# Halves of the second softmax's product with x, eight array places for batches 2 and 3, and two M blocks split ahead of the product

## The reference

```python
def _attn_ref(x, state):                     # x [4, 8, 512, 64], state [4, 8, 32, 64]
    scores = x @ state.T / 8;   a  = softmax(scores);   xread = a @ state
    scores2 = state @ x.T / 8;  a2 = softmax(scores2);  sread = a2 @ x
    return concat([xread, sread], axis=2)    # 544 rows of 64 for each head
# rows to tokens: 4 * 544 = 2176 tokens of 512
def _moe_ref(x, w_in, w_out):                # 512 -> 2048 -> 512
    h = x @ w_in;  return (h * tanh(softplus(h))) @ w_out
def _moe2_ref(x, emb, tau, w1, w2):          # 8 experts, one for each token
    expert = argmax(cosine(x, emb) / tau);  gate = softmax(...)[expert]
    return gate * (relu(x @ w1[expert]) @ w2[expert])
```

## Time and profile before

| | us |
|---|---|
| median of 3 runs | 708.38 |
| lowest and highest | 705.73 and 714.18 |
| the profiled execution, its own time | 706.29 |
| its span | 704.5 |
| TensorE matmul busy in the span | 655.5 |
| VectorE and ScalarE busy | 443.0 and 385.8 |

### The profile page before, as it was taken

How to read it: one execution, slowest core, us unless ns; L and a number is a source line. 1 busy time by engine, 2 the same in 40 slices (tenths; PEclk the granted TensorE clock), 3 DMA queues, 4 the chain that set the end, 5 groups by cost and what they waited for, 6 DMA issues and landing times. The chain is left out here.

```text
span 704.5 us, 12383 instructions
## 1 busy us (share of the span) xinstructions
PE 655.5 (93%) x4142; PEld 512.6 (73%) x4143; DVE 443.0 (63%) x687; ACT 385.8 (55%) x501; POOL 51.6 (7%) x75
## 2 busy tenths in 40 slices
PE   7889979999889999899999888989999999999995
PEld 5667756687667787676588776768888888888884
DVE  6899889888658699576668446472722452272261
ACT  2788679785747787476867333262612442262250
POOL 2000000000200002000002013000001010010101
PEclk9999999999999999999999989999999999999999
DMA  8804443000823002233001612372531261154140
GB/s 245 234 32 132 146 143 120 1 2 25 276 62 120 0 2 86 97 120 120 0 1 61 224 41 81 126 263 91 203 111 45 83 230 34 45 189 139 45 149 5
DMA packets 35350, 72.72 MB, mean 103 GB/s; under 512 B 5699, under 2 KB 5699, under 8 KB 35312
## 3 DMA queue, kind: packets, MB, share of 16 engines
q1 hardware_dynamic: 27728, 56.93, 25.0%
q0 software_dynamic: 3040, 9.13, 3.3%
q10 hardware_dynamic: 4544, 6.14, 3.0%
HBM read 60.92 MB, written 12.16 MB: 104 GB/s over the span
## 5 line engine op out<-in xcount | busy, mean ns | idle before, releaser
L613 PE MATMUL PS<-WH,gh 128*128 128x512 f32 x256 | 103.3, 404 | 0.8 <-DVE gl L1401 0.8
L613 PE MATMUL PS<-WH,gl 128*128 128x512 f32 x256 | 101.0, 395 | 0.0
L613 PE MATMUL PS<-WL,gh 128*128 128x512 f32 x256 | 101.0, 394 | 0.0
L1066 ACT ACTIVATE hh<-PS 128x512 fp32r<-128x512 f32 x42 | 22.9, 595 | 97.5 <-PE PS L717 94.6
L736 PE MATMUL PS<-WH,hh 128*128 (+1 forms) x168 | 69.2, 412 | 3.9 <-DVE hl L1487 2.6
L1477 DVE TENSOR_TENSOR WL<-raw,WH 128x1024 f32 (+1 forms) x48 | 56.3, 1221 | 25.3 <-ACT WH L1046 25.2
L736 PE MATMUL PS<-WH,hl 128*128 (+1 forms) x168 | 67.3, 400 | 0.0
L736 PE MATMUL PS<-WL,hh 128*128 (+1 forms) x168 | 66.9, 398 | 0.0
L1378 DVE SCALAR_TENSOR_TENSOR qq<-ww,PS 128x1024 f32<-128x1024 f32 (+1 forms) x35 | 41.5, 1186 | 36.4 <-ACT ww L963 36.3
L979 ACT ACTIVATE ww<-ww,cst 128x1024 f32<-128x1024 f32 (+1 forms) x35 | 39.4, 1127 | 41.7 <-DVE ww L1383 41.7
L613 PEld LDWEIGHTS PS<-WH,gh 128*128 128x128 f32 x256 | 48.2, 188 | 18.8 <-issue 7.5
(11 more groups left out here) (252 smaller groups left out, 1278.3 us busy)
## 6 DMA issues: line engine op xcount, KB each, us to landing
raw<-in_w SPq DMA_DIRECT2D x48, 512.0 KB, 4.7
raw<-in_w_in SPq DMA_DIRECT2D x36, 512.0 KB, 5.0
yg<-by_expert ACTq DMA_DIRECT2D x22, 260.0 KB, 3.0
raw<-in_w_out SPq DMA_DIRECT2D x8, 512.0 KB, 4.8
by_expert<-junk SPq DMA_DIRECT2D x1, 2080.0 KB, 10.1
wr<-in_w_in SPq DMA_DIRECT2D x4, 512.0 KB, 10.4
x_0a<-in_x SPq DMA_DIRECT2D x8, 128.0 KB, 2.9
x_0b<-in_x SPq DMA_DIRECT2D x8, 128.0 KB, 3.3
```

Source lines behind the costliest of these rows:

```text
L613: mm = pe.matmul(PS[:, 2 + t, :], a[:, v % 2, e, t * P:t * P + P], w[:, 8 + p, e * 512:e * 512 + 512], start=(p == 0 and e == 0 and i == 0 ...
L1066: a.activation(hh[:, 4 * j:4 * j + 4, :], PS[:, 3 + j, :].rearrange("p (k m) -> p k m", k=4), ACT.Copy).then_inc(hh_rdy, 1)
```

## The change

Lines of the diff, cut to its core. `sread` gets a second argument, a slice of its 32 pairs (g, t).

```diff
+        def sr_bank(b, g):
+            return 6 if b < 2 else 6 + g
+        def sh_upto(b):
+            return (4, 8, 10, 12)[b]
+        def bv_upto(b):
+            return (2, 4, 10, 16)[b]
@@ SP
-            for r in range(12, RING["w", 2 * NB, 0]):
+            for r in range(12, RING["w", 2 * NB + 2, 0]):
                 stream(r)
             load_x(3)
@@ TensorE, M
-                if nb == 1 and c > 1:
-                    pe.wait_ge(shn_rdy, 2 * c + 2)
                 if nb == 2 and c > 1:
-                    pe.wait_ge(sh_e, 4 * c + 4)
+                    pe.wait_ge(sh_e, sh_upto(c))
@@ TensorE, sread
-            def sread(b):
+            def sread(b, part):
                 pe.wait_ge(e2d_rdy, b + 1)
                 if b > 1:
-                    pe.wait_ge(m_lo, NB * b + 1)
+                    pe.wait_ge(m_lo, NB * b + 2)
...
+                order = [(g, t) for g in range(HG) for t in range(16)] if b < 2 else [(g, t) for t in range(16) for g in range(HG)]
+                for g, t in order[part]:
+                    for j in range(4):
+                        q = j if b < 2 else j ^ g
+                        mm = pe.matmul(PS[32 * q:32 * q + 32, sr_bank(b, g), D * g:D * g + D], E2D[b][32 * j:32 * j + 32, g, 32 * t:32 * t + 32],
+                                       X2[b % 2][t // 8][32 * j:32 * j + 32, g, t % 8, :],
+                                       start=(t == 0), stop=(t == 15))
@@ TensorE, order of steps (ahead = the first 16 pairs, behind = the other 16)
                     if p == 4:
+                        if c == 1:
+                            sread(1, behind)
                         route_k(c - 1)
-                if c < 3 and p >= 5:
+                    if p == 6:
+                        sread(c + 1, ahead)
+                    if p == 7:
+                        sread_turned(c + 1)
+                if c > 1 and p == 0:
+                    M(c, 3)
+                if c == 0 and p >= 5 or c in (1, 2) and p == 5:
                     M(c + 1, p - 5)
...
                     if p == 3 and c == 1:
-                        sread(1)
+                        sread(1, ahead)
                     if p == 5 and c > 0:
-                        sread(c + 1)
+                        M(c + 1, 1)
                     if p == 6 and c > 0:
-                        sread_turned(c + 1)
+                        sread(c + 1, behind)
                     if p == 7:
-                        M(c + 1, 3)
+                        M(c + 1, 3 if c == 0 else 2)
@@ ScalarE, step n of chunk c
+                if n == 7 and c in (1, 2):        # between mish_a and mish_hi
+                    M_hi(c + 1, 0)
...
-                if kind == "m" and n < 3 and c > 0:
+                if kind == "m" and (n < 3 and c == 1 or n == 2 and c > 1):
                     M_hi(c, n + 1)
+                if c > 1 and n == 1:
+                    sread_out(c)                  # before: at the end of step 0
                 mish_b(u)
+                if n == 7 and c in (1, 2):
+                    M_hi(c + 1, 1)
                 if done >= 0 and n == 1:
                     y_out(done)
+                    if c > 1:
+                        M_hi(c, 2)
@@ VectorE, soft_5
+                    v.reciprocal(r2[:, b % 2, 3, 0:1], r2[:, b % 2, 2, 0:1]).then_inc(bv, 1)
+                    for j in range(4):
+                        q = j ^ 1
+                        v.reciprocal(r2[32 * q:32 * q + 32, b % 2, 3, 1:2], r2[32 * j:32 * j + 32, b % 2, 2, 1:2]).then_inc(bv, 1)
@@ VectorE, step n of chunk c
                 mish_q(u)
+                if n == 7 and c in (1, 2):
+                    M_lo(c + 1, 0)
                 if SEQ[u - 1][0] == "m":
                     mish_lo(u - 1)
-                if kind == "m" and n < 3 and c > 0:
+                if kind == "m" and (n < 3 and c == 1 or n == 2 and c > 1):
                     M_lo(c, n + 1)
...
                 mish_r(u)
+                if n == 7 and c in (1, 2):
+                    M_lo(c + 1, 1)
+                if n == 1 and c > 1:
+                    M_lo(c, 2)
                 if done >= 0 and n == 1:
                     y_out(done)
                 mish_g(u)
+                if n == 0 and c > 1:
+                    sread_scale(c)                # before: at the end of step 7
...
-                    if n == 5 and c == 1:
-                        soft_5(2)
-                    if n == 6 and c == 2:
-                        soft_5(3)
+                    if n == 5 and c > 0:
+                        soft_5(c + 1)
```

More of the change, by code:

```diff
@@ L363, in _ @@
             load_x(2)
-            for r in range(12, RING["w", 2 * NB, 0]):
+            for r in range(12, RING["w", 2 * NB + 2, 0]):
                 stream(r)
             load_x(3)
-            for r in range(RING["w", 2 * NB, 0], len(STREAM)):
+            for r in range(RING["w", 2 * NB + 2, 0], len(STREAM)):
                 stream(r)
@@ L520, in sread @@
                     pe.wait_ge(sc_e, 4)
[L521 to L527, removed]
+                order = [(g, t) for g in range(HG) for t in range(16)] if b < 2 else [(g, t) for t in range(16) for g in range(HG)]
[5 more added lines that the diff above has]
+                                       start=(t == 0), stop=(t == 15))
+                if part.stop is None:
+                    mm.then_inc(sr_mm, 1)
             def sread_turned(b):
@@ L584, in HB @@
             def HB(p):
-                pe.wait_ge(sh_e, 4 * B)
+                pe.wait_ge(sh_e, sh_upto(B - 1))
                 pe.wait_ge(m_lo, NB * B)
@@ L744, in _ @@
             t0 = (0, 0)
+            whole, ahead, behind = slice(0, None), slice(0, 16), slice(16, None)
             H_first()
@@ L758, in _ @@
                     if p == 4:
-                        sread(0)
+                        sread(0, whole)
                 if c in (1, 2):
@@ L928, in sread_out @@
                 for h in range(2):
-                    for g in range(HG):
-                        a.activation(sh[D * h:D * h + D, 2 * g:2 * g + 2, NS * b:NS * b + NS], ps[:, g, :, h if g == 0 else 1 - h, :],
+                    if b < 2:
+                        for g in range(HG):
+                            a.activation(sh[D * h:D * h + D, 2 * g:2 * g + 2, NS * b:NS * b + NS], ps[:, g, :, h if g == 0 else 1 - h, :],
+                                         ACT.Copy).then_inc(sh_e, 1)
+                    else:
+                        a.activation(sh[D * h:D * h + D, :, NS * b:NS * b + NS].rearrange("p (g q) n -> p g q n", g=HG), ps[:, :, :, h, :],
                                      ACT.Copy).then_inc(sh_e, 1)
@@ L1166, in _ @@
                         exp_2(c + 1)
-                if kind == "m" and c > 1 and n == 0:
-                    sread_out(c)
             mish_hi(LAST)
@@ L1336, in sread_scale @@
                 dve.wait_ge(sr_mm, b + 1)
[L1337 removed]
+                dve.wait_ge(bv, bv_upto(b))
                 if b > 0:
@@ L1609, in _ @@
                 mish_q(u)
+                if n == 7 and c in (1, 2):
+                    M_lo(c + 1, 0)
                 if SEQ[u - 1][0] == "m":
                     mish_lo(u - 1)
-                if kind == "m" and n < 3 and c > 0:
+                if kind == "m" and (n < 3 and c == 1 or n == 2 and c > 1):
                     M_lo(c, n + 1)
-                if n == 7 and c in (1, 2):
-                    M_lo(c + 1, 0)
                 if c == 1 and n == 0:
```

16 lines of the change are left out of this document (7 added, 9 removed).

## The result

| | before | after |
|---|---|---|
| median of 18 runs each, us | 711.38 | 704.76 |
| lowest and highest | 705.73, 714.30 | 702.18, 708.38 |
| profiled execution: own time, span | 706.29, 704.5 | 703.76, 702.0 |
| its mean granted clock | 0.986 | 0.976 |

The ratio is 0.9921, 95% interval 0.9903 to 0.9939: 4.3 to 6.9 us faster (6.6 between the medians), where 9.5 were forecast, and 704.76 lies above the range of 693.5 to 702.5. The kernel before also has a higher median here, 711.4, than the 708.4 of its first three runs.

What follows compares the result with a forecast made beforehand. TensorE was taken as the bound, its matmuls busy for 93% of the span. Batches 1, 2 and 3 gain 1.4 + 5.1 + 3.0 = 9.5 us; 707.3 - 9.5 = 697.8, forecast 697.5 us, range 693.5 to 702.5.

Steps and rivals of the forecast that it cites:

- The base: Starting time of the kernel before: 707.3 us, middle of four known executions; the profiled one was 706.29 us.
- Part 1: Products of batches 1 to 3 in halves around long work: all four issue stalls go; batch 1 gains 1.4 us.
- the stall in H: Issue stall of 1.24 us in H behind batch 2's product; forecast to go with the halving.
- Part 2: Products of batches 2 and 3 on eight places instead of four: 1.9 us a product, 1.7 us gained for each batch.
- Rival (c): In the product's halves, weight loads wait for neighbours on the same rows: 5.2 us a half, 714.5 us; chance 0.04.
- Part 3: M(b,1) ahead of the product: batch 2's 2.8 us of waiting become 2.6; batch 2 in all gains 5.1 us.
- Part 4: soft_5(3) one step earlier with five reciprocals on VectorE: H(23) 1.7 us late, a 1.03 us wait goes; batch 3 gains 3.0.
- a worked list of 3.2: Batch 3's gain in us from working three lists step by step; the terms summed to 2.5, and 3.0 was taken.
- Part 5: M rows of batch 2 loaded ahead of x of batch 3, at chunk 0's end: worth nothing by itself.
- the choice between the two figures: Forecast total: 697.5 us taken between 696.8 (from the profiled execution) and 697.8 (from the 707.3 middle).
- (a): Rival: VectorE, full from 243 to 283 us, gives part back; gain 5 us, 702.5 us; chance 0.15.
- (d): Rival: chunks' gain lost later in gathers and routing clock dips, or an unforeseen wait undoes the halves; 704 us; chance 0.06.

Runs made afterwards that it cites:

- whole_moved: four_places with the products of batches 1 to 3 whole again, all moves kept; median 709.6 us, ratio to before 0.9982.
- eight_whole: The kernel before with eight places alone for batches 2 and 3 (with reciprocals and copies), product whole and where it was; median 710.7 us, ratio 1.0016.
- b1_loads: The kernel before with only batch 1's product in halves and the new load order; median 710.7 us, ratio 0.9984.
- four_places: The changed kernel with batches 2 and 3 back on four places, one reciprocal and the small copies, halves and moves kept; median 703.1 us, ratio to before 0.9885.
- loads_old: The changed kernel with the M rows of batch 2 sent behind x of batch 3 again; median 705.6 us, ratio to before 0.9906.
- b1_halves: The kernel before with only batch 1's product in halves and its old load order; median 709.8 us, ratio 0.9995.

## Why the forecast was wrong, point by point

- **The base: wrong by 4 us, the largest single share.** The forecast started from 707.3, "the middle of the four known executions", one of them the profiled 706.29 at a clock of 0.986. The median of 18 runs is 711.4, and the mean clock of 52 others is 0.978. The fit puts the kernel before at 707.2 us for a clock of 0.986, so for the profiled execution the clock explains most of the distance. For the other three it is not on record, and why the middle of the four lay so low stays open. With 711.4 the same 9.5 us would have given 701.9, inside the range; with 707.3 the true gain of 6.6 would have given 700.7, inside it as well. It took both errors to miss.
- **Part 1, the halves: right, but for the stall in H.** The stalls of the three halved products went, 1.4 us in batch 1 were 1.36. The fourth stall, 1.24 us in H, was put down to the halves and goes without them too: whole_moved and eight_whole have none. That stalls come from blocks of 256 instructions being eaten in half the time that they need holds in each variant: whole products at full clock stall (before, eight_whole, whole_moved, batch 0 of after), halves never do, and neither does the whole product at half clock (b1_loads). The trace's own packets say the same. In the profile before, TensorE's list went on by 4860 records while 19 packets of 16 KB came on the instruction queue (from 74.5 to 389.7 us), 256 records for each. Around the product of batch 2 such packets start at 195.33 and 199.05 us, and TensorE starts again 2.7 and 2.9 us behind them; those of one whole product lie 3.5 to 4.0 us apart in before and eight_whole. After the change the nearest to the products of batches 1 to 3 lie 4.8 us and more apart, and only batch 0's whole product has two at 3.7. The Trainium skill, Runtime: NRT & Kernel Launch, section Instruction fetch mechanics, calls a border mostly hidden; 1.3 to 1.4 us for each of the three products, between whole_moved and four_places (the last by the estimate for the dip), say that for this stream it is not.
- **Part 2, the places: right mechanism, wrong size.** 1.4 us for a half where 0.9 to 1.1 were taken, so 1.1 us for a batch and not 1.7; short by 0.6 twice. The bounds, 1.8 to 3.6 us a product, held 2.8. I took the value near M's rate and should have weighed that a record of the product carries an eighth of M's columns. Rival (c), weight loads one by one, is out: its half of 5.2 us met 1.40. The rule of the Trainium skill, TensorE: Matmul & The Clock Gate, section Part 3: Packing small matmuls — row/col tiling, that weight loads overlap running matmuls only where the row groups differ, doesn't agree with this trace. The rows of before could have told: on four places too each weight load follows a matmul on its own rows, and a round of four passes in 56 ns, though a load is recorded with 105.
- **Part 3, M ahead of the product: right in size.** The waits were 1.6 and 0.8 us for 1.7 and 0.9. The order alone is worth 1.4 to 2 us in batch 2, most of it the stall in H. Batch 2 gave 4.4 for 5.1, and 0.6 of the missing 0.7 is that of Part 2.
- **Part 4, VectorE: the sign right, the size not.** The reciprocals cost 0.18 each, not 0.1; the 0.1 was the distance to the transpose behind the one reciprocal, and the row that it was read from has a duration of 0.17. With their starts and ends the four cost 0.86 us for 0.4. H(23) waited 2.0, not 1.7. Batch 3 brought 1.6 for 3.0: 0.6 from the places, 0.3 from H, and 0.5 because I took 3.0 between a sum of 2.5 and a worked list of 3.2; the sum was the better of the two. The cost was avoidable: with the reciprocals at their use and `soft_5(3)` at its old step batch 3 gives 3.6.
- **Part 5, the loads: the number nearly right, the reason wrong.** 0.2 us, but not because nothing waits: with the old order M(2,0) waits 1.5 to 1.9 us for its rows (loads_old, b1_halves), and nearly all of it comes out of the waits for splits behind it.
- **What is left.** The chunks brought 7.3 us, the medians 6.6 and the levels at equal clock 6.4 +- 0.6. The 0.7 to 0.9 between lie in the routing and the expert tiles or in the 0.7 us by which two profiles of one kernel differ; this stays open.

From 697.5 to 704.76 are 7.3 us: 4.1 of the base, 0.3 of the choice between the two figures (697.8 and 697.5), 2.9 of the gain. So the steps that failed are the base of 707.3 us, the 1.9 us for a product on eight places (2.8 measured), and the 3.0 us for batch 3 (1.6). Of the rivals, (a) came nearest in what happened: VectorE gave part back, once and not in every place. The 704 us of (d) lie nearest to 704.76, by chance: the gain was neither lost behind the chunks nor undone by a wait.

## What to carry to other kernels

Before forecasting from one profiled execution, compare its mean granted clock with that of other executions; here 0.01 of clock was worth 4 us, more than half of the change. The dense run of small matmuls of this kernel was limited by its instructions twice, by the fetching of blocks and by the rate of records, so split such a run around long work first and look for more places second. An operation added to a full VectorE belongs at the place where its result is used: there the addition and five small reciprocals of batch 3 cost no wait of TensorE, and ahead of the splits they cost 1.06 us. One such product is left: that of batch 0 still stalls for 1.18 us, and no run here splits it.

## What the runs showed of the hardware

- Over the chunks of the kernel before, instructions came in packets of 16 KB, one for each 256 of TensorE's records. A stream that took 256 records in 1.8 us stalled for 1.0 to 1.7 us in each whole product; at half clock, 3.4 us for 256, it didn't (b1_loads).
- Records of small matmuls: 128 pairs of weight load and matmul (32 x 32 tiles) pass in 1.2 us with 32 moving columns, on four places or eight; with 64 columns in 1.4 us on eight places and 1.9 on four. Tiles that share rows in pairs gained by eight places, 1.40 us a half for 1.92.
- A reciprocal of 32 x 1 costs VectorE 0.18 us in a row of four, as much as the 0.17 of one with 128 x 1.
- The granted clock falls to 0.50 in places that differ between executions: over the same 30 us of chunk 0 the mean was 1.00 and 0.94 in two profiles of the kernel before and 0.89 in that after, though TensorE had stood still for 3.6 to 4.1 us up to 103 us in all three. One dip costs some 1.7 us by the two windows of whole_moved, 1.55 by batch 3 of loads_old against that of after (99.13 for 97.58), and next to nothing on the product of b1_loads.
